# Written-out expert loops on two engines, and later tiles that remake chunk 7 instead of chunks 3 and 7

## The reference

```python
# 1: attention over a window of 128 keys and 4 sinks: 4 batches x 8 heads x 768 x 64
# 2: mixture of experts over N = 3072 rows of D = 512, E = 8 experts, F = 1024
do_compute = (x @ w_skip) > 0
xc = x[do_compute]
e_idx = np.argmax(xc @ w_gate, axis=1)          # one expert for each row
for e in range(E):
    mask = e_idx == e
    h = np.maximum(xc[mask] @ w1[e], 0.0)
    y[mask] = gate_w[mask, None] * (h @ w2[e])
out[do_compute] = xc + y
# 3: (relu(x @ w_in) ** 2) @ w_out, d_ff = 2048
```

## Time and profile before

| | us |
|---|---|
| median of 3 runs | 921.86 (921.29 to 923.27) |
| the profiled execution | 920.97 |
| its span, first to last instruction | 919.5 |
| TensorE busy | 896.5 (97%) |
| VectorE busy | 471.4 (51%) |
| ScalarE busy | 422.1 (46%) |
| mean granted clock of TensorE | 0.997 |

### The profile page before, as it was taken

One profiled execution on the slowest core, in us unless ns is written; L12 is line 12 of the kernel. 1 busy time (PEld: TensorE's weight loads), 2 busy tenths in 40 slices (PEclk: granted clock), 3 DMA queues, 4 the chain that ended last, 5 costly groups with the idle time before them and its releaser, 6 DMA issues.

```text
span 919.5 us, 16966 instructions
## 1 busy us (share of the span) xinstructions
PE 896.5 (97%) x5152; PEld 728.7 (79%) x5153; DVE 471.4 (51%) x1418; ACT 422.1 (46%) x971; POOL 81.4 (9%) x147
## 2 busy tenths in 40 slices
PE   7999999989999998999999999999999999999998
PEld 5878777767888886788888888888888888888886
DVE  5787899885777667663242224222422332243224
ACT  7888999855666666552232113211322221232123
POOL 3112222223111111100000000000000000000000
PEclk9999999999999999999999999999999999999999
DMA  5556665285666778630012003100400040004001
GB/s 200 171 167 205 229 229 173 83 291 208 248 224 240 246 280 309 250 70 0 1 52 41 1 1 74 18 0 0 91 0 0 0 91 0 0 0 91 0 0 46
DMA packets 87364, 99.52 MB, mean 108 GB/s; under 512 B 56093, under 2 KB 56221, under 8 KB 87312
## 3 DMA queue, kind: packets, MB, share of 16 engines
q1 hardware_dynamic: 81168, 83.34, 28.6%
q0 software_dynamic: 6000, 15.49, 4.8%
q10 hardware_dynamic: 144, 0.07, 0.0%
HBM read 77.72 MB, written 25.56 MB: 112 GB/s over the span
## 4 chain that ended last, share of the span: by engine, by line
PE 88%; issue 3%; ACT 3%; DMA 2%; DVE 2%; ACTq 1%; DVEq 0%; SPq 0%; POOLq 0%
PE bank L1158 29%; PE bank L1144 28%; PE bank L1056 6%; PE bank L1037 6%; PE bank L896 4%; PE bank L951 4%; PE bank L924 4%; DMA w_raw<-in_weights 2%; PE bank L962 1%; PE bank L1045 1%; ACT prob L682 1%; PE bank L976 1%; ACT w_hi L792 1%; PE bank L944 1%; PE bank L1029 1%
## 5 line engine op out<-in xcount | busy, mean ns | idle before, releaser
L1527 DVE TENSOR_TENSOR g<-relu_c 128x512 f32<-128x512 f32 x96 | 66.5, 692 | 340.7 <-ACT relu_c L839 340.6
L839 ACT ACTIVATE relu_c<-bank 128x512 f32<-128x512 f32 x96 | 57.4, 598 | 371.6 <-PE bank L1144 371.6
L1144 PE MATMUL bank<-x_hi,w_lo 128*128 128x512 f32 x384 | 149.5, 389 | 0.7 <-DVE x_lo L1514 0.7
L1158 PE MATMUL bank<-w_hi,g_lo 128*128 128x512 f32 x384 | 150.1, 391 | 0.0
L1158 PE MATMUL bank<-w_hi,g_hi 128*128 128x512 f32 x384 | 149.4, 389 | 0.0
L1158 PE MATMUL bank<-w_lo,g_hi 128*128 128x512 f32 x384 | 149.4, 389 | 0.0
L1144 PE MATMUL bank<-x_lo,w_hi 128*128 128x512 f32 x384 | 149.4, 389 | 0.0
L1144 PE MATMUL bank<-x_hi,w_hi 128*128 128x512 f32 x384 | 149.4, 389 | 0.0
L682 ACT ACTIVATE prob<-score,neg_max 128x264 f32<-128x264 f32 (+1 forms) x192 | 94.0, 496 | 14.1 <-DVE neg_max L1220 14.0
L1486 DVE TENSOR_TENSOR w_lo<-w_raw,w_hi x70 | 82.0, 1221 | 22.6 <-ACT w_hi L792 15.9
L1158 PEld LDWEIGHTS bank<-w_hi,g_lo 128*128 128x128 f32 x384 | 72.1, 188 | 17.2 <-DVE g_lo L1534 2.5
(11 more groups left out here) (150 smaller groups left out, 1275.7 us busy)
## 6 DMA issues: line engine op xcount, KB each, us to landing
w_raw<-in_weights SPq DMA_DIRECT2D x80, 512.0 KB, 5.1
k_in<-in_kT SPq DMA_DIRECT2D x24, 264.0 KB
q_in<-in_qT SPq DMA_DIRECT2D x24, 256.0 KB, 3.2
v_in<-in_v SPq DMA_DIRECT2D x24, 256.0 KB
x_rows<-x_row SPq DMA_DIRECT2D x24, 256.0 KB
x_row<-x_rows SPq DMA_DIRECT2D x96, 64.0 KB, 2.5
out<-w_raw SPq DMA_DIRECT2D x12, 512.0 KB, 2.9
x_res<-routed POOLq DMA_DIRECT2D x15, 260.0 KB, 3.1
```

The lines of the kernel that those rows point to most:

```text
L839: eng.activation(relu_c[:, f % 2, :], hc_ps[f % 2][:, :], ACT.Relu).then_inc(s_crelu, 1)
L1144: ins = eng.matmul(hc_ps[f % 2][:, :], w[f // UNIT][:, f % UNIT, wcols], x[:, c, :], start=(c == 0 and n == 0), stop=(c == DC - 1 and n == 2))
L1158: ins = eng.matmul(yc_ps[s][:, :], gg[:, f % 2, s * P:(s + 1) * P], w[f // UNIT][:, f % UNIT, DM:CH], start=(f == 0 and n == 0), stop=(f = ...
L1527: eng.tensor_tensor(g[:, f % 2, :], relu_c[:, f % 2, :], relu_c[:, f % 2, :], ALU.mult).then_inc(s_cg, 1)
```

## The change

In later tiles both groups make chunk 7 once more, and chunk 3 is left alone. SP's load of chunk 3 then waits, like those of 0, 1, 2, 4, 5 and 6, only for its own `w_lo`; in the last expert the wait for the scatter and the loading of the third layer's first rows move from ahead of chunk 3 to ahead of chunk 7. ScalarE's waits on VectorE become stricter, since it writes a `w_hi` chunk that VectorE has just read: a later tile's group 0 waits for all parts of the tile before, and its group 1 for group 0's part of the same tile. On ScalarE and VectorE all eight experts are written out; each takes the `end` of the expert before as its `first` and loads only its `end`, inside the tile loop of the expert before. TensorE keeps its loop, and SP its own, which was written out already and loads both values.

```diff
--- before.py
+++ after.py
@@ -365,7 +365,7 @@
         def group(k, later):
 
             first, size = ((0, HEAD), (HEAD, UNIT - HEAD))[k]
-            return size - later * (size - 1), later * (size - 1) + first
+            return size - later * (size - 1), later * (UNIT - 1 - first) + first
 
         def is_later(eng, n, first):
 
@@ -395,6 +395,16 @@
                     e = m * 2 + slot
                     first, end = expert_tiles(eng, e)
                     body(e, slot, first, end)
+
+        def end_of(eng, e):
+
+            return eng.value_load(table[0:1, E + e:E + e + 1], min_val=1, max_val=MAX_TILES)
+
+        def each_expert_ahead(eng, body):
+
+            first, end = 0, end_of(eng, 0)
+            for e in range(E):
+                first, end = end, body(e, e % 2, first, end)
 
         def all_tiles(eng):
             return eng.value_load(table[0:1, 2 * E - 1:2 * E], min_val=E + 1, max_val=MAX_TILES)
@@ -513,16 +523,13 @@
 
                 made = parts_ahead(e, first)
                 for f in range(UNIT):
-                    if e == E - 1 and f == HEAD - 1:
+                    if e == E - 1 and f == UNIT - 1:
 
                         eng.wait_ge(s_bscatter, tiles * 16)
                         close(eng)
                         load_first_x()
-                    if f == HEAD - 1 or f == UNIT - 1:
-                        last = parts_ahead(e + 1, end) - (UNIT - HEAD if f < HEAD else 0)
-                        if f < HEAD:
-                            last = is_later(eng, end - 1, first) * (UNIT - HEAD - 1) + last
-                        eng.wait_ge(s_wlo, last)
+                    if f == UNIT - 1:
+                        eng.wait_ge(s_wlo, parts_ahead(e + 1, end))
                         close(eng)
                     else:
                         eng.wait_ge(s_wlo, made + f + 1)
@@ -782,9 +789,8 @@
                     eng.wait_ge(s_whi, made)
                     close(eng)
 
-                    before_is_later = is_later(eng, n, first + 1) if k == 0 else 0
                     lower = parts_ahead(e, n) + later * (UNIT - 2)
-                    eng.wait_ge(s_wlo, lower if k == 1 else lower - (UNIT - HEAD) + before_is_later * (UNIT - HEAD - 1))
+                    eng.wait_ge(s_wlo, lower + later if k == 1 else lower - (UNIT - HEAD) + later * (UNIT - HEAD))
                     close(eng)
                     chunk_loaded(e + 1, k * HEAD)
                     with eng.Fori(0, size) as c:
@@ -798,16 +804,19 @@
                 h_upper(n, 0)
                 if at_once:
                     chunks(0)
+                next_end = end_of(eng, e + 1) if e + 1 < E else None
                 relu_b(n, 1)
                 x_upper(n + 1)
                 h_upper(n, 1)
 
                 eng.wait_ge(s_by, n + 1)
                 chunks(1)
+                return next_end
 
             def expert(e, slot, first, end):
-                with eng.Fori(1 if isinstance(e, int) and e == 0 else first, end) as n:
-                    tile(e, n, slot, first)
+                with eng.Fori(1 if e == 0 else first, end) as n:
+                    next_end = tile(e, n, slot, first)
+                return next_end
             def last_output():
 
                 eng.wait_ge(s_pv, ITEMS * TILES)
@@ -820,7 +829,7 @@
             first_tile()
             eng.wait_ge(s_table, 1)
             tiles = all_tiles(eng)
-            each_expert(eng, expert)
+            each_expert_ahead(eng, expert)
 
             eng.wait_ge(s_brow, tiles + 1)
             close(eng)
```

## The result

| | before | after |
|---|---|---|
| median | 922.26 us (6 runs, 921.29 to 923.27) | 925.28 us (6 runs, 924.08 to 926.67) |
| ratio | | 1.0031, 95% interval 1.0017 to 1.0046 |
| profiled execution, its span | 920.97, 919.5 | 924.41, 922.9 |

The change made the kernel 3.0 us slower, 0.3%. I had forecast 2.95 us faster, 918.9, and my range for 8 in 10 ended at 922.4.

What follows compares the result with a forecast made beforehand. TensorE, busy 97% of the span, was taken to bound the kernel. From the profiled 920.97: -0.4 (loads), -3.3 (loops), +0.75 (added wait), 0 (start) = -2.95, so 918.0, as median 918.9; 8 in 10: 916.4 to 922.4.

Steps and rivals of the forecast that it cites:

- the added wait: Tiles 4, 6, 8, 10, 14: ScalarE waits for VectorE's chunk 7, costing 0.15 us each, 0.75 in all.
- What bounds the kernel: Whole kernel: TensorE, busy 97% of the span; in the expert stage only its 4.4 us of waits for relu count.
- my 7 us of what the stage can give back: Expert stage: 4.4 us of waits, 0.9 of restarts and 1.6 of clock, about 7 us.
- My forecast of tile 13: Tile 13's turn of `h` was to come at 362.05 in place of 365.49, 3.4 us earlier; 3.3 taken.
- My 0.22 for a restart: Turn of `h` in TensorE: each turn that had to wait costs 0.22 us beyond its gap.
- the clock's part of tile 12 to 13: Behind tile 12's wait the clock fell to 1.2 GHz, costing 1.57 us, taken as saved.
- The start of the stage: Tiles 0 to 2: four chunks loaded early delay POOL's last paddings 1.5 us, inside the slack; cost 0, bounds 0 and 1.5.
- Rival 2: Start of the stage: padding lands 3 us later, tile 2's second layer waits 1.5 us; 920.4 us, chance 0.15.
- The loops written out, in tiles 12 and 13: VectorE 1.4 us earlier at tile 11 brings the weights earlier for tiles 12 and 13; gain 3.3 us, bounds 0.4 and 5.0.
- rival 1: Tiles 12 and 13: the DMA takes the shift back, leaving a gain of 0.4 us; 921.8 us, chance 0.15.
- The loads of chunks 3 to 6: Tile 3 gets chunk 3 sooner, a gain of 0.4 us; tiles 5, 7, 9, 11, 12 and 13 gain 0.
- Rival 3: Written-out code stalls on instruction fetch at branches back in six tiles; 923.7 at 0.8 us each, 927.9 at 1.5; chance 0.12.

Runs made afterwards that it cites:

- experiment 1: Changed kernel, but SP holds expert 0's chunk 3 and those behind it until tile 3's rows have landed: 922.07 us, ratio to before 1.0006.
- experiment 5: Changed kernel with expert 0's chunks 3 to 7 held until tile 3's rows landed and later tiles' group 0 making chunk 6: 921.41 us, ratio 0.9991.
- Experiment 8: Changed kernel, loading half the columns of chunks 0 to 3 for expert 7 and the third layer's first half: 922.44 us, ratio to before 1.0012.
- experiment 3: Kernel before with only ScalarE's and VectorE's loops written out; groups, loads and waits as before: 921.86 us, ratio 0.9989.
- Experiment 2: Changed kernel, but group 0 of later tiles makes chunk 6 in place of chunk 7: 924.71 us, ratio to before 1.0033.
- experiment 4: Changed kernel's chunks, SP loads and ScalarE waits, but with the loops of the kernel before: 925.83 us, ratio to before 1.0035.
- Experiment 6: Changed kernel, but SP holds expert 0's chunk 3 and those behind it only until POOL's padding has landed: 925.11 us, ratio to before 1.0031.
- experiment 7: Changed kernel, loading half the columns of chunks 3 to 6 for expert 2, moved into tiles 0 and 1: 922.84 us, ratio to before 0.9999.

## Why the prediction was wrong, point by point

**Two terms of the sum failed.** The median was to fall by 2.95 us and rose by 3.0. In the profiled execution the difference of the spans is 6.3 us from my sum: 2.8 at the start (2.37 for -0.4), 2.7 in tiles 12 and 13 (-0.62 for -3.3), 0.8 from ahead of the experts, nothing in the added wait. Either of the first two alone would have taken nearly all of the forecast gain away. That the kernel became slower is the start's doing, as experiments 1 and 5 show.

**What bounds the kernel** was read rightly in its places: the two waits in tiles 12 and 13 are where the stage can gain. But my 7 us of what the stage can give back counted both in full. Experiment 8 shows that 0.9 us in each belongs to ScalarE. My forecast of tile 13 had this chain, 13.15 us long, because I put ScalarE's second group 4.2 us behind the turn; it starts 4.5 behind, and the chain is 13.4. My 0.22 for a restart was mis-sized as well: it came from mixing the chain of work with TensorE's timeline. In the timeline alone tile 14 followed 12.39 behind tile 13, so a restart is 0.06, and the clock's part of tile 12 to 13 is 1.7 and not 1.57.

**The start of the stage is the first step that failed.** I gave the four moved chunks a cost of 0 (bounds 0 and 1.5). It was 2.4 us in the profiled execution, and 2.3 and 3.9 by the times of experiments 1 and 5. I had the cause and the queue right, and erred in the size of the delay and in who waits for it.
- I let a third to a half of the 5.2 us of DMA fall on the last paddings. Here are POOL's last padding write of the changed kernel and the windows behind it (length, busy by engine, PEclk, DMA share, GB/s):

```profile
L386 POOL DMA_DIRECT2D routed<-pad_row x1: 542/542/542, 213.3 to 213.3; - x1
...
DMA to landing us min/median/max: 8.4/8.4/8.4
```

```profile
216.00:220.00 4.00, 4.00 (x19) 3.16 (x18) 3.05 (x5) 1.48 (x2) 0.00 (x0) 1.00 1.02 415
```

  Before, it took 4.7, so it took 3.7 us longer, where I had 1.5. The engines stayed saturated up to about 221 us, where before they had been through at about 215.
- I checked one consumer behind POOL's scatter, `y_row` and the second layer of tile 2, and found 1.7 us of slack. The next instruction on POOL's queue was the load of tile 3's rows, which TensorE needs ahead of that layer:

```profile
223.11 1.01 POOL L622 DMA_INDIRECT x_rows<-y_row,y_of  x1 [9.27 <-issue]
224.13 0.56 POOL L632 DMA_DIRECT2D x_res<-routed  x1
224.70 0.57 POOL L660 IOTA column<- 128x512 int32 x1
225.69 0.56 POOL L647 DMA_DIRECT2D x_raw<-routed  x1 [0.42 <-issue]
```

```profile
228.91 0.66 PE L1038 MATMUL bank<-ident,x_raw 128*128 128x128 f32 x4 [2.58 <-DMA x_raw<-routed]
```

  The scatter of the earlier trace rows came 4.0 us later (0.8 of it from ahead of the stage), the rows landed at 228.9, and TensorE stood 2.58 us. Before, they had landed at 224.6, and the turn's weight load began at 225.2. That is 0.6 us of slack, and I had not looked. The kept traces agree on this: counted from tile 0's turn the rows land at 28.8 to 29.1 us where the loads are not moved or are held (before, experiments 1, 3 and 5), and at 31.6 to 32.5 where they are moved whole (changed, experiments 2, 4, 6 and 8).
- I had no clock in this term. Behind the wait for the rows it stayed up in the changed kernel and in experiments 2 and 6, and it fell in experiments 4 and 8, which costs 1.7 us more.
- Rival 2 named this place, with padding 3 us late and a cost of 1.5. Its mechanism was the nearest, one instruction off; its time, 920.4, was not near.

**The loops written out, in tiles 12 and 13, are the second step that failed.** I took 3.3 us for them; experiment 3 measured 1.0 (from 2.2 faster to 0.2 slower). They do what I said on the engines. VectorE's idle time at a boundary fell from 2.15 us to 0.56:

```profile
336.53 4.63 DVE L1495 TENSOR_TENSOR w_lo<-w_raw,w_hi  x4 [0.56 <-ACT w_hi L798]
```

Counted from tile 11's turn its group began 1.6 us earlier. But the last chunk's load did not: counted from that turn it went out at 2.41 us in place of 4.00 and landed at 10.24 in place of 10.63, since it took 7.8 us in place of the 6.63 of the earlier trace rows:

```profile
L449 SPq DMA_DIRECT2D w_raw<-in_weights x1: 328/328/328, 341.3 to 341.3; - x1
...
DMA to landing us min/median/max: 7.8/7.8/7.8
```

I had taken the duration of the transfer along with its start. In the kernel before, POOL's scatter and `x_res` went out at -1.95 and -0.91 and had landed at 0.69 and 2.10, so they were nearly done when the weights began at 0.59. Now the weights begin at -1.00 and all share the engines: the scatter takes 5.5 us in place of 2.6, `x_res` 6.6 in place of 3.0. Of 1.6 us 0.4 were left. This is rival 1, which priced tiles 12 and 13 at 0.4. With the wait still at 2.48 the clock fell again, as these two windows show, so the 1.57 for it was not saved either:

```profile
353.00:355.00 2.00, 1.18 (x5) 1.19 (x6) 2.00 (x3) 0.80 (x3) 0.56 (x2) 0.66 0.95 309
355.00:357.00 2.00, 2.00 (x6) 1.52 (x6) 1.22 (x2) 0.57 (x1) 0.00 (x0) 0.50 0.96 333
```

Tiles 12 and 13 gave 0.62 us in place of 3.3. That this comes so near to rival 1's price is luck of this execution, as the other traces show (us; the load of the fourth chunk is counted from tile 11's turn):

| trace | load out, landed (took) | wait in tile 12 | tile 11 to 14 | low clock behind |
|---|---|---|---|---|
| before | 4.0, 10.6 (6.6) | 2.52 | 42.90 | tile 12 |
| 4, old loops | 4.0, 10.9 (6.9) | 2.82 | 43.23 | tile 12 |
| changed | 2.4, 10.2 (7.8) | 2.48 | 42.36 | tile 12 |
| 1 | 2.4, 9.6 (7.1) | 1.79 | 42.87 | tile 13 |
| 2 | 2.3, 9.1 (6.8) | 1.23 | 39.37 | none |
| 3 | 2.4, 10.4 (8.0) | 2.57 | 42.58 | tile 12 |
| 5 | 2.3, 10.1 (7.9) | 2.28 | 40.93 | none |
| 6 | 2.4, 9.0 (6.6) | 1.25 | 42.35 | tile 13 |
| 7 | 2.4, 10.6 (8.2) | 2.83 | 42.83 | tile 12 |
| 8, half the data | 2.4, 6.6 (4.2) | 0.90 | 39.34 | none |

In the seven with written-out loops and whole chunks the load goes out 1.6 to 1.7 us earlier than before and lands 0.1 to 1.6 earlier, 0.8 on average. The stretch is 1.0 us shorter on average than the 42.90 before, which fits the 1.0 of experiment 3. Experiment 2's execution had what I forecast for all: a wait of 1.2 us, no low clock, 3.5 us gained. My step took the best case for the usual one. The clock is no surer: it fell behind a wait of 1.96 us (experiment 1, tile 13) and not behind one of 2.28 (experiment 5, tile 12).

**The added wait** was right in place and size: 0.66 us from tile 3 to 11 and 0.08 in tile 14, where I had 0.15 in each of the five later tiles. Its mechanism is plain in ScalarE's timeline from tile 3 to 4, beside the earlier trace rows:

```profile
250.34 1.06 ACT L798 ACTIVATE w_hi<-w_raw  x1 [2.47 <-DVE w_lo L1495]
251.30 0.58 ACT L759 ACTIVATE h_b<-bank 128x512 f32<-128x512 f32 x1
```

VectorE's last part ended at 249.94 and ScalarE began 0.40 behind it, as worked out; relu no longer has a moment to spare.

**The loads of chunks 3 to 6** in tile 3: the wait of 0.19 is gone, as forecast. With a restart of 0.06 it was worth 0.25 and not 0.4.

**Rival 3**, written-out code, is refuted by experiment 3, whose interval ends at 0.2 us slower. The rule of the Trainium skill that I set beside it (Runtime: NRT & Kernel Launch, Instruction fetch mechanics) warned more of the old loop. No row shown here has such a stall. I had priced one branch over the outer loop at 0.4, VectorE's 2.57 us at tile 9 less 2.15 at tile 11. In the changed kernel, where no outer loop is left, the two are 0.93 and 0.56, so the 0.4 is still there and was not the branch; what it is stays open.

## What to carry to other kernels

Where the DMA engines are saturated, a load that is issued earlier need not land earlier by the same amount (1.6 us became 0.8 on average here), and what is in flight beside it lands later (`x_res` took 6.6 us in place of 3.0): move its bytes in the sum, not its landing time. Before a load is moved up, list what lands in the stretch that it moves into, follow the queue behind each of these to every instruction, and compare the slack of the next one as well as of the first. An order that looks like a needless wait may be what keeps a transfer out of the way of a more urgent one. And read a wait under load from several executions: in seven kernels that are nearly alike there, the one in tile 12 was 1.2 to 2.8 us long.

## What was not expected of the hardware

Experiment 6 is the surprise. With the engines saturated the order of issue did little: 2 MB issued ahead of the padding made the padding take 8.4 us in place of 4.7 and left tile 3's rows at 3.2; the same 2 MB issued behind it left the padding at 5.0 and made the rows take 6.4. TensorE waited 2.6 and 2.4 us. Holding the loads until the rows had landed took the wait away; halving their bytes took away half of the rows' delay.

Which of tile 12's transfers takes most from the fourth chunk was not separated. Single executions of one kernel lie up to 6 us apart, and the clock is a part of that. The ten profiled executions have none to two stretches of the experts in which the granted clock is at its 1.2 GHz level, each behind one of TensorE's waits and worth about 1.7 us: none in experiments 2 and 5, two in experiments 4 and 7. Of the 29 runs of the kernel before that experiments 5, 6 and 8 were compared with, the seven with a mean granted clock of 1.000 took 919.5 to 921.3 us, the other 22 took 920.8 to 925.1. What decides whether a given wait is followed by such a stretch stays open.
